# Six units of 512 tokens across batches in the time-mix and channel gate, in place of eight half batches of 384

## The reference, cut to what matters

```python
x_prev = np.concatenate([zeros((B, 1, D)), x[:, :-1, :]], axis=1)
xk = mu_k * x + (1.0 - mu_k) * x_prev
xr = mu_r * x + (1.0 - mu_r) * x_prev
k = np.maximum(xk @ w_k, 0.0)            # 384 -> 1024
v = k * k @ w_v                          # 1024 -> 384
r = 1.0 / (1.0 + np.exp(-(xr @ w_r)))    # 384 -> 384
return r * v
```

## Time and profile before

| what | value |
|---|---|
| median of 3 runs | 729.55 us (729.25 to 729.72) |
| time of the profiled execution | 729.78 us |
| its span, first to last instruction | 728.0 us |
| PE matmul, busy share | 99% |
| DVE / ACT / POOL, busy share | 65% / 46% / 27% |
| last stage on the chain of waits | 487.96 to 725.10 us |

### The profile page before, as it was taken

One profiled execution on the slowest core, in us unless ns is written; L12 is line 12 of the kernel. 1 busy time (PEld: TensorE's weight loads), 2 busy tenths in 40 slices (PEclk: granted clock), 3 DMA queues, 4 the chain that ended last, 5 costly groups with the idle time before them and its releaser, 6 DMA issues.

```text
span 728.0 us, 13834 instructions
## 1 busy us (share of the span) xinstructions
PE 722.9 (99%) x4539; PEld 717.2 (99%) x4539; DVE 472.2 (65%) x1298; ACT 331.6 (46%) x953; POOL 198.9 (27%) x348
## 2 busy tenths in 40 slices
PE   8999999999999999999999999999999999999998
PEld 7999999999999999999999999999999999999998
DVE  7988888865988865888883412446447365373561
ACT  5876544433544442544442332426346364373550
POOL 3876564333243432334332530310000000000000
PEclk9999999999999999999999999999999999999999
DMA  9965436542335554243531323010011010110000
GB/s 211 224 147 89 86 52 121 77 68 70 52 54 78 104 81 86 39 53 61 113 56 33 94 91 130 33 44 23 32 55 44 33 43 26 50 43 32 11 23 32
DMA packets 210347, 50.90 MB, mean 70 GB/s; under 512 B 190512, under 2 KB 207472, under 8 KB 210288
## 3 DMA queue, kind: packets, MB, share of 16 engines
q1 hardware_dynamic: 207008, 45.05, 31.1%
q0 software_dynamic: 1280, 4.72, 1.8%
q10 hardware_dynamic: 2000, 0.41, 0.3%
HBM read 37.17 MB, written 12.98 MB: 69 GB/s over the span
## 4 chain that ended last, share of the span: by engine, by line
PE 98%; DVE 1%; issue 0%; ACT 0%; POOL 0%; DVEq 0%; POOLq 0%
PE bank L834 21%; PE bank L850 21%; PE bank L938 14%; PE bank L916 14%; PE bank L925 5%; PE bank L746 5%; PE bank L714 4%; PE bank L822 4%; PE bank L787 3%; PE bank L751 2%; PE bank L744 2%; PE bank L709 1%; PE bank L671 1%; PE bank L803 1%; PE bank L722 1%; PE bank L874 0%
## 5 line engine op out<-in xcount | busy, mean ns | idle before, releaser
L1035 ACT ACTIVATE hid_hi<-bank 128x384 fp32r<-128x384 f32 x96 | 47.2, 492 | 115.8 <-PE bank L834 115.7
L1312 DVE SCALAR_TENSOR_TENSOR hid_lo<-bank,hid_hi 128x384 fp32r<-128x384 f32 x96 | 53.2, 554 | 65.2 <-ACT hid_hi L1035 64.0
L1137 ACT ACTIVATE relu_k<-bank 128x384 f32<-128x384 f32 x64 | 31.5, 491 | 106.0 <-PE bank L916 86.2
L834 PE MATMUL bank<-u_hi,wch_hi 128*128 128x384 f32 x288 | 72.2, 358 | 0.0
L834 PE MATMUL bank<-u_lo,wch_hi 128*128 128x384 f32 x288 | 66.3, 338 | 0.0
L850 PE MATMUL bank<-hid_lo,wch_hi 128*128 128x384 f32 x288 | 65.5, 335 | 0.0
L834 PE MATMUL bank<-u_hi,wch_lo 128*128 128x384 f32 x288 | 65.5, 335 | 0.0
L850 PE MATMUL bank<-hid_hi,wch_hi 128*128 128x384 f32 x288 | 65.4, 334 | 0.0
L850 PE MATMUL bank<-hid_hi,wch_lo 128*128 128x384 f32 x288 | 65.4, 334 | 0.0
L1452 DVE TENSOR_TENSOR x_half<-bank,x_half 128x384 f32<-128x384 f32 (+2 forms) x25 | 13.4, 541 | 77.5 <-PE bank L938 75.3
L587 POOL TENSOR_SCALAR_AFFINE_SELECT relu_k<-relu_k 128x256 f32<-128x256 f32 x72 | 29.3, 407 | 111.5 <-ACT relu_k L1017 111.5
(11 more groups left out here) (142 smaller groups left out, 1831.5 us busy)
## 6 DMA issues: line engine op xcount, KB each, us to landing
w_raw<-in_moe_w_ch SPq DMA_DIRECT2D x12, 384.0 KB, 3.5
out<-x_half SPq DMA_DIRECT2D x23, 192.0 KB, 1.9
vt<-in_v SPq DMA_DIRECT2D x48, 72.0 KB, 2.3
x_scratch<-x_sum SPq DMA_DIRECT2D x18, 192.0 KB, 2.1
x_sum<-x_scratch SPq DMA_DIRECT2D x72, 48.0 KB, 2.2
qka<-in_alpha SPq DMA_DIRECT2D x49, 48.0 KB, 2.2
qka<-in_k SPq DMA_DIRECT2D x49, 48.0 KB, 2.2
qka<-in_q SPq DMA_DIRECT2D x49, 48.0 KB, 2.3
```

The source lines that it names most:

```text
L834: mm = nc.tensor.matmul(dst, ch1_w(a, n % KC, jj), u[c][:, n % KC, half * HT:(half + 1) * HT], start=(n == 0), stop=(n == 3 * KC - 1))
L1035: nc.scalar.activation(dst, b_ring[t % 2][:, 0:HT], func).then_inc(tile_hi, 1)
L1312: ins = nc.vector.scalar_tensor_tensor(dst, src, 0.0, hi, ALU.max, ALU.subtract)
```

## The change

The stage now goes over six units of 512 tokens (`UT`, number `un`). A unit is two thirds of 256 tokens, and since a batch has three thirds, units 1 and 4 cross from one batch to the next. `third_of(un, k)` gives the batch and the third. The loads are two DMAs a unit, each with its own token ahead; where a third begins a batch, that token's column is set to zero, by DVE for unit 0 and by POOL for the others, and ACT waits for it (`first_zeroed`).

- `ff_up` makes 8 hidden tiles of 128 by 512 a unit, with the same 9 matmuls a tile. `receptance` and `ff_down` make 4 token tiles a unit, in place of 3 a half. Tile `t = 4 * un + m` takes bank `t % 3` of the same three banks.
- All elementwise operations of ACT and DVE between x2 and the hidden tiles are 512 wide in place of 384. Gates and outputs stay 384 wide; there are four buffers of each.
- Unit 0's mixes: only the three of kind 0 are made in mixer slots, 21 to 27 (slots 15 to 27 for all six before). Its kind 1 mixes are made beside its own hidden tiles, as for every other unit.
- No loops: all engines' programs of the stage are written out.
- Some buffers lie elsewhere: the second `x2_in` in `x_sum` (its first load waits until all weights are split), the second relu buffer in `decays`, the second `mixed` in `qkd`, the kind 1 mixes partly in `hid`.

The diff, cut to its core:

```diff
+    UT = 512
+    THIRD = S // 3
+    UNIT_TILES = UT // P
+    NU = B * S // UT
...
-    MIX_SLOT = SLOTS - 4 * KC - 1
+    MIX_SLOT = SLOTS - 2 * KC - 1
...
+            def load_x2(un):
+                if un >= 2:
+                    sp.wait_ge(mixed_ready, 2 * KC * (un - 1))
+                for k in range(2):
+                    b, third = third_of(un, k)
...
+                    prev = min(third, 1)
+                    sp.dma_start(x2_in[un % 2][:, :, k, 1 - prev:THIRD + 1],
+                                 x2_dram[b, :, third * THIRD - prev:(third + 1) * THIRD].rearrange("(c p) t -> p c t", p=P))\
+                      .then_inc(x2_loaded[un % 2], 16)
...
+            load_x2(0)
+            sp.wait_ge(w_lo_ready, lo_count(NALL))
+            load_x2(1)
+            for un in range(NU):
+                if un + 2 < NU:
+                    load_x2(un + 2)
+                store_out(un)
...
+            pool.wait_ge(w_lo_ready, lo_count(NALL))
+            for un in range(1, NU):
+                for k in range(2):
+                    if third_of(un, k)[1] == 0:
+                        if un >= 2:
+                            pool.wait_ge(mixed_ready, 2 * KC * (un - 1))
+                        nc.gpsimd.memset(x2_in[un % 2][:, :, k, 0:1], 0.0).then_inc(first_zeroed, 1)
...
-                dst = b_ring[j % 2][:, 0:HT]
+                dst = b_ring[j % 2][:, 0:UT]
...
+            def receptance(un, m):
+                t = UNIT_TILES * un + m
+                pe.wait_ge(gate_ready, t + 1)
                 for n in range(3 * KC):
                     a, c = PASSES[n // KC]
...
+                    mm = nc.tensor.matmul(b_acc[t % 3][:, 0:DM], mix_out[1][a][n % KC][:, m * P:(m + 1) * P],
+                                          wr_w(c, n % KC), start=(n == 0), stop=(n == 3 * KC - 1))
...
+            for un in range(NU):
+                pe.wait_ge(mix_lo, 2 * KC * un + KC)
+                for j in range(NF):
+                    ff_up(un, j)
+                pe.wait_ge(mix_lo, 2 * KC * (un + 1))
...
+                for m in range(UNIT_TILES):
+                    receptance(un, m)
...
+                for m in range(UNIT_TILES):
+                    ff_down(un, m)
...
+            def unit_pass(un):
                 for j in range(NF + 1):
...
+                    mix_for_gate(un, j)
+                if un + 1 < NU:
+                    for n in range(KC + 1):
+                        mix_for_up(un + 1, n)
+                if un == 0:
+                    act.wait_ge(x2_stored[0], 16 * B)
+                for m in range(UNIT_TILES):
+                    t = UNIT_TILES * un + m
+                    act.wait_ge(r_done, t + 1)
+                    if t > 0:
+                        act.wait_ge(y_ready, t)
+                    nc.scalar.activation(gate[m], b_acc[t % 3][:, 0:DM], ACT.Sigmoid).then_inc(gate_ready, 1)
```

More of the change, by code:

```diff
@@ L97, in attention_mixer_channel_mix @@
         x2_half = [sb(f"x2_half{n}", [P, KC, HT]) for n in range(2)]
-        qka = [sb(f"qka{n}", [P, KC * (HT + 1)]) for n in range(2)]
+        QKA = KC * (HT + 1)
+        qka_words = sb("qka_words", [P, 2 * QKA])
+        qka = [qka_words[:, n * QKA:(n + 1) * QKA] for n in range(2)]
         vt = [sb(f"vt{n}", [P, DM]) for n in range(2)]
@@ L238, in attention_mixer_channel_mix @@
         y_ready = sem("y_ready")
-        y_stored = [sem(f"y_stored{n}") for n in range(TM)]
+        y_stored = [sem(f"y_stored{n}") for n in range(UNIT_TILES)]
         y_free = sem("y_free")
@@ L483, in _ @@
                 load_piece(n)
[L486 to L501, removed]
+            def load_x2(un):
[3 more added lines that the diff above has]
+                    b, third = third_of(un, k)
+                    if third < 2:
+                        sp.wait_ge(x2_stored[0], 16 * b + 16)
+                    if third > 0:
+                        sp.wait_ge(x2_tile_stored, 16 * b + 16)
+                        sp.wait_ge(x2_stored[1], 16 * b + 16)
+                    prev = min(third, 1)
+                    sp.dma_start(x2_in[un % 2][:, :, k, 1 - prev:THIRD + 1],
+                                 x2_dram[b, :, third * THIRD - prev:(third + 1) * THIRD].rearrange("(c p) t -> p c t", p=P))\
+                      .then_inc(x2_loaded[un % 2], 16)
@@ L502, in store_out @@
+            def store_out(un):
+                for m in range(UNIT_TILES):
+                    n = UNIT_TILES * un + m
+                    sp.wait_ge(y_ready, n + 4)
+                    store_rows(sp, un, m, LAST_COLS[0] if n == UNIT_TILES * NU - 1 else slice(0, DM))
+                for m in range(UNIT_TILES):
+                    n = UNIT_TILES * un + m
+                    sp.wait_ge(y_stored[m], 16 * (un + 1 + (n == UNIT_TILES * NU - 1)))
                 sp.sem_inc(y_free, 1)
             sp.wait_ge(consts_v, 6)
-            for half in range(2):
-                load_x2(0, half)
@@ L943, in _ @@
             pe.wait_ge(w_lo_ready, lo_count(WK_END))
[L944 to L950, removed]
+            for un in range(NU):
[4 more added lines that the diff above has]
+                if un == 0:
                     pe.wait_ge(w_lo_ready, lo_count(WR_END))
-                    for m in range(TM):
-                        receptance(hn, half, m)
+                    pe.wait_ge(acc_read, 2 * KC * B + 1)
+                for m in range(UNIT_TILES):
+                    receptance(un, m)
+                if un == 0:
                     pe.wait_ge(w_lo_ready, lo_count(NALL))
-                    for m in range(TM):
-                        ff_down(hn, m)
+                for m in range(UNIT_TILES):
+                    ff_down(un, m)
         @block.scalar
@@ L1056, in tile_second, with scale_prev @@
                     down_high(b, 2 * s - 1)
-            def scale_prev(hn, half, n):
+            def scale_prev(un, n):
                 kind, c = divmod(n, KC)
-                if not isinstance(hn, int) or 2 * KC * hn + n >= 2:
-                    act.wait_ge(mix_lo, 2 * KC * hn + n - 1)
+                if 2 * KC * un + n >= 2:
+                    act.wait_ge(mix_lo, 2 * KC * un + n - 1)
                 if n == 0:
-                    act.wait_ge(x2_loaded[half], 8 * (hn - half) + 16)
-                nc.scalar.activation(mixed[:, n % 2, :], x2_in[half][:, c, 0:HT], ACT.Copy,
-                                     scale=omu[:, kind, c:c + 1]).then_inc(scaled, 1)
@@ L1069, in mix_high @@
-            def mix_high(hn, half, n):
-                kind, c = divmod(n, KC)
[L1071 to L1080, removed]
@@ L1082, in mix_for_gate @@
-            def mix_for_gate(hn, half, j):
-                if j < 2 * KC:
[L1085 to L1091, removed]
+                    act.wait_ge(x2_loaded[un % 2], 32 * (un // 2 + 1))
+                    zeroed = sum(third_of(w, k)[1] == 0 for w in range(1, un + 1) for k in range(2))
@@ new lines, in scale_prev, with mix_high @@
+                    if zeroed:
+                        act.wait_ge(first_zeroed, zeroed)
+                nc.scalar.activation(mixed_ring[n % 2].rearrange("p (k t) -> p k t", k=2), x2_in[un % 2][:, c, :, 0:THIRD],
+                                     ACT.Copy, scale=omu[:, kind, c:c + 1]).then_inc(scaled, 1)
+            def mix_high(un, n):
+                kind, c = divmod(n, KC)
+                act.wait_ge(mixed_ready, 2 * KC * un + n + 1)
+                nc.scalar.activation(mix_out[kind][0][c], mixed_ring[n % 2], ACT.Copy).then_inc(mix_hi, 1)
@@ L1138, in half_pass @@
                             .then_inc(relu_ready, 1)
                     if j >= 1:
-                        act.wait_ge(k2_ready, NF * hn + j)
-                        nc.scalar.activation(k2[0][:, j - 1, :], relu_k[:, (j - 1) % 2, :], ACT.Copy)\
+                        act.wait_ge(k2_ready, NF * un + j)
+                        nc.scalar.activation(k2[0][:, j - 1, :], relu_ring[(j - 1) % 2], ACT.Copy)\
                             .then_inc(k2_hi, 1)
-                    if not first:
-                        mix_for_gate(hn, half, j)
@@ L1145, in half_pass @@
[L1145 to L1156, removed]
@@ L1163, in _ @@
+            for un in range(NU):
+                unit_pass(un)
+            act.wait_ge(y_ready, UNIT_TILES * NU + 4)
+            store_rows(act, NU - 1, UNIT_TILES - 1, LAST_COLS[1])
         @block.vector
@@ L1443, in half_pass @@
-                mix_next(nxt, 1 - half)
-                dve.wait_ge(x2_tile_stored, 16 * B)
-                dve.wait_ge(x2_stored[1], 16 * B)
-                for m in range(TM):
-                    dve.wait_ge(gate_ready, TM * hn + m + 4)
-                    dve.wait_ge(v_done, TM * hn + m + 1)
-                    dve.wait_ge(y_free, hn + 1)
-                    last = nxt is None and m == TM - 1
-                    for cols in LAST_COLS if last else (slice(0, DM),):
-                        nc.vector.tensor_tensor(y_out[:, m, cols], bank[m][:, cols], gate[:, m, cols], ALU.mult)\
```

(23 more changed lines are left out.)

126 lines of the change are left out of this document (63 added, 63 removed).

## The result

The changed kernel takes 751.37 us (median of 6, 751.00 to 751.94) against 729.44 us of the kernel before (6 runs, 729.25 to 729.72). The ratio is 1.030, 95% interval 1.029 to 1.031: slower by 21.9 us. The profiled execution took 751.94 us, 22.2 more than the one of before.

What follows compares the result with a forecast made beforehand. TensorE, busy 99% of the span, was taken as the bound, with any new wait added in full. Against 729.78 us, - 1.9 + 16.1 + 1.4 gave 745 us; range 739 to 748, to 752 with one clock fall.

Steps and rivals of the forecast that it cites:

- rival B: In the last stage's pauses TensorE's clock falls: one fall 748 us, 14%; several 12%, with one in each of five units 760.
- step 1: In `ff_up`, 432 matmuls of 512 columns replace 576 of 384: 1.9 us less.
- Step 2: In `receptance`, the fourth tile waits for the first tile's gate to free its bank: 16.1 us, plus 1.4 in unit 0.
- Step 3: ACT and DVE work beside `ff_up` stays hidden, with 0.15 us to spare a tile: nothing added.
- Steps 4 and 5: At the stage's start unit 0's last mix, and later the loads, stores and zeros, come in time: nothing added.
- Rival A: The fourth `receptance` tile does not wait, so only the gain of the wide matmuls is left: 727.6 us, 4%.

## Why the prediction was right, and where it fell short

The direction, the place and the mechanism were right: 745 us was forecast, in a range of 739 to 752, and 751.4 came. The missing 6.4 us come from one term, rival B, which I had kept out of the sum: the falls cost 7.3 us, while the delays came out 1.0 lower than forecast and step 1 saved 0.3 less. That 751.4 still lies under the upper end of 752 is partly luck. That end was worked out for one fall at 3 us or a little more; four came, at about half that price.

- **Step 1** gave 2.04 us a tile and 1.9 us in all; the chain has 16.38 / 8 = 2.05 and 1.6. In most of the timeline of `ff_up` three matmuls of 512 columns take 0.68 us from start to start, 0.2267 each, as the line through 256 and 384 columns had it. The 215.8 ns, an estimate by the formula for an isolated matmul on the Trainium skill's page "TensorE: Matmul & The Clock Gate", section "Back-to-back issue gap", does not fit this stream of fp32r weight loads and matmuls, at 512 columns no more than at 384. (By it the total would have been 432 x 10.9 ns = 4.7 us lower, not the 4 that the prediction has.)
- **Step 2**, the gate: 7.50 us was worked out, 7.37 measured. Relu 0.60 for 0.61, high part 0.63 for 0.65, scale 0.72 for 0.74. The growth by width from the earlier trace rows held. The restart was put too high, 0.39 against 0.32 (0.05 from the gate to the tile, and 1.83 instead of 1.56 for the tile): the weight load of 0.19 us does not stand in the open in full. In the trace the load and the first matmul are both shown from 0.05 us after the gate. Together 3.01 a unit instead of 3.21. Unit 0 had 1.43 more, 1.4 predicted (511.01: the table load in the chain itself). 16.5 us instead of 17.5.
- **The clock** was the step that failed. I took "no row shows a fall" as evidence against it, but in the kernel before TensorE had no pause in which it could have shown. With several falls at 12% I gave 760 us. Several is what happened, in four pauses of five, at a lower price than the start of the kernel had suggested: 3 us each were put, for half of a low stretch of 6 us, and 1.6 came three times and 2.5 once. The low stretches here were 3.4 us long three times, and the one of 6.8 us began while TensorE still stood, so that about 5.5 us of it were matmuls; each fall cost about half of the low time in which TensorE worked. Whether the start of the kernel runs at the lower level at all stays open: the granted clock reads 1.00 there and 0.50 in the falls. The section on idle gaps of the Trainium skill's page "TensorE: Matmul & The Clock Gate" ("Why this matters for your kernels") pointed the right way; the runs with the pause filled show that it was the pauses.
- **Step 3**: relu of tile 7 started the moment `ff_up` ended (550.24), so ACT and DVE kept up, and TensorE had no wait in `ff_up`.
- **Steps 4 and 5** cost nothing. The last mix of unit 0 and POOL's work:

```profile
485.57 0.69 DVE L1400 TENSOR_TENSOR x_lo<-mixed,x_hi 128x512 fp32r<-128x512 f32 x1
```

```profile
473.35 1.85 POOL L562 TENSOR_TENSOR wch_lo<-x_sum,wch_hi 128x768 fp32r<-128x768 f32 x1 [1.27 <-ACT wch_hi L992]
...
490.43 0.12 POOL L684 MEMSET x_sum<- 128x3 f32 x1
```

The low part ended at 486.26, before `ff_up` began at 487.60; the last weight split at 475.20; the zeros for unit 1 were written at 490.43, and ACT read them at 505.9. That written-out programs cost nothing, the run of the kernel before with its loops written out shows.
- **Rival A**, no stall at 727.6 us, is what two of the experiments are: 1.4 and 1.6 us under before.

## What to carry to other kernels

When more tiles than there are banks go through one stage, look for the first tile that needs a bank of the same pass and ask where its release stands in the program of the engine that gives it, not whether that engine is busy. A kernel at 99% of one engine has no slack for a wait, but the release may be had for nothing by moving one instruction ahead of work with a later due time. And price a new pause of TensorE with the clock as part of it before calling it the sum: a fall cost 1.6 to 2.5 us here, on top of a delay of 3.

## What the runs showed of the hardware that was not expected

- The clock's answer to a pause is not sharp in its length. In the profiled executions none of five pauses of 1.1 to 1.2 us had a fall behind it, one of four of 1.8 did, the one of 2.6 did, three of four of 2.75 did, the one of 3.2 did not, and the eight from 3.6 us on all did. These are single executions, and others of the same kernel differ: the pause of 2.6 us had a fall in two executions of four. In the changed kernel itself the granted clock was 0.989 in three executions (751.64 to 751.94 us) and 0.991 in the other three (751.00 to 751.10). What decides between equal pauses stays open; no run varied anything that would tell them apart.
- A fall can begin in the pause or after it. In unit 0 of the changed kernel the granted clock is 0.77 already from 511 to 512, while TensorE stands until 512.85. In unit 4 it is still 1.00 from 688 to 689, with TensorE at work since 687.69, and 0.51 from 689 to 690. So there the fourth tile lost only 2.15 - 1.83 = 0.3 us and `ff_down` 1.3, while in unit 2 the tile lost 1.2 and `ff_down` 0.4, with the same pause.
